# One block, three stages: Strassen's seven products for the channel mixing of an attention and mixer block

## The reference

```python
def _moe2_ref(x, w_tok1, w_tok2, w_ch1, w_ch2):      # the part that is changed
    xt = x.transpose(0, 2, 1)
    h = np.maximum(xt @ w_tok1, 0.0) @ w_tok2        # token mixing, 576 -> 256 -> 576
    u = x + h.transpose(0, 2, 1)
    h2 = np.maximum(u @ w_ch1, 0.0) @ w_ch2          # channel mixing, 512 -> 1536 -> 512
    return (u + h2).astype(np.float32)

def reference(...):
    attn_out = _attn_ref(...)                        # 8 heads, windows of 32 keys, plain or dilated by 4
    x = attn_out.transpose(0, 2, 1, 3).reshape(B, S, H * D)
    x = _moe_ref(x=x, ...)                           # shift mix, relu squared, sigmoid gate
    return _moe2_ref(x=x, ...)
```

## Time and profile before

| what | value |
|---|---|
| median of 3 runs | 696.34 us (695.63 to 697.08) |
| the profiled execution, span from first to last instruction | 694.4 us |
| the profiled execution's own time | not given apart from its span; the median lies 1.9 us above the span |
| TensorE busy (PE) | 686.7 us, 99% |
| VectorE (DVE), ScalarE (ACT), GpSimd (POOL) busy | 362.6, 230.6 and 201.7 us |
| mean granted clock of TensorE | 0.997 |
| first matmul of the mixer | 335.6 us |
| DMA | 181493 packets, 47.23 MB |

### The profile page before, as it was taken

How to read it: one execution, slowest core, us unless ns; L and a number is a source line. 1 busy time by engine, 2 the same in 40 slices (tenths; PEclk the granted TensorE clock), 3 DMA queues, 4 the chain that set the end, 5 groups by cost and what they waited for, 6 DMA issues and landing times.

```text
span 694.4 us, 15537 instructions
## 1 busy us (share of the span) xinstructions
PE 686.7 (99%) x6377; PEld 613.1 (88%) x6377; DVE 362.6 (52%) x635; ACT 230.6 (33%) x516; POOL 201.7 (29%) x249
## 2 busy tenths in 40 slices
PE   8999999999999999999999999999999999999997
PEld 7879999999999999999888879888788888888886
DVE  5579877676868668586752145221462125311121
ACT  4573653536353554546421122111231122111110
POOL 6574646546464645453072000000000000000000
PEclk9999999999999999999999999999999999999999
DMA  9972243233423331343630310403122221300011
GB/s 202 227 183 47 52 80 79 44 65 71 88 43 65 56 79 38 82 68 119 246 58 14 59 43 34 68 13 64 61 35 34 43 35 60 64 6 0 1 61 30
DMA packets 181493, 47.23 MB, mean 68 GB/s; under 512 B 168360, under 2 KB 173872, under 8 KB 181424
## 3 DMA queue, kind: packets, MB, share of 16 engines
q1 hardware_dynamic: 172448, 40.82, 26.9%
q10 hardware_dynamic: 8976, 5.43, 3.1%
HBM read 31.53 MB, written 4.72 MB: 52 GB/s over the span
## 4 chain that ended last, share of the span: by engine, by line
PE 97%; ACT 1%; DVE 1%; POOL 0%; issue 0%; DVEq 0%; POOLq 0%; ACTq 0%
PE bank L968 13%; PE bank L970 12%; PE bank L969 12%; PE tq L968 8%; PE tq L970 8%; PE tq L969 8%; PE s L1574 4%; PE s L1573 4%; PE s L1572 4%; PE bank L1573 3%; PE bank L1574 3%; PE bank L1572 3%; PE bank L844 3%; PE bank L1023 2%; PE s L632 2%; PE bank L768 1%
## 5 line engine op out<-in xcount | busy, mean ns | idle before, releaser
L1564 DVE SCALAR_TENSOR_TENSOR h_lo<-bank,h_hi 128x512 fp32r<-128x512 f32 (+1 forms) x30 | 18.9, 637 | 100.7 <-ACT h_hi L1558 100.6
L1564 DVE SCALAR_TENSOR_TENSOR h_lo<-tq,h_hi 128x512 fp32r<-128x512 f32 (+1 forms) x30 | 18.9, 636 | 99.0 <-ACT h_hi L1558 99.0
L1063 POOL TENSOR_TENSOR k_lo<-kr,k_hi 128x288 fp32r<-128x288 f32 x64 | 55.2, 866 | 25.6 <-ACT k_hi L1059 25.5
L1105 DVE RECIPROCAL rg<-rg 128x288 f32<-128x288 f32 x32 | 61.4, 1921 | 0.0
L1558 ACT ACTIVATE h_hi<-tq 128x512 fp32r<-128x512 f32 (+1 forms) x30 | 16.7, 556 | 118.7 <-PE bank L1574 97.0
L1558 ACT ACTIVATE h_hi<-bank 128x512 fp32r<-128x512 f32 (+1 forms) x30 | 16.7, 556 | 118.0 <-PE bank L1574 93.4
L968 PE MATMUL bank<-k_hi,WV_hi 128*128 128x288 f32 x184 | 55.5, 301 | 0.0
L969 PE MATMUL bank<-k_hi,WV_lo 128*128 128x288 f32 x184 | 54.3, 295 | 0.0
L970 PE MATMUL bank<-k_lo,WV_hi 128*128 128x288 f32 x184 | 54.1, 294 | 0.0
L1574 PE MATMUL s<-C_hi,h_lo 128*128 128x512 f32 x120 | 47.6, 396 | 0.0
L1572 PE MATMUL s<-C_hi,h_hi 128*128 128x512 f32 x120 | 47.1, 393 | 0.3 <-DVE urows L1601 0.3
(11 more groups left out here) (239 smaller groups left out, 1982.8 us busy)
## 6 DMA issues: line engine op xcount, KB each, us to landing
C_raw<-in_moe_w_ch SPq DMA_DIRECT2D x6, 1024.0 KB, 10.9
urows<-blocks SPq DMA_DIRECT2D x64, 64.0 KB, 2.1
out_x<-urows SPq DMA_DIRECT2D x16, 256.0 KB, 2.0
vt<-in_v SPq DMA_DIRECT2D x70, 48.0 KB
qraw<-in_q SPq DMA_DIRECT2D x128, 24.0 KB, 1.9
kraw<-in_k SPq DMA_DIRECT2D x128, 24.0 KB, 2.0
xraw<-blocks SPq DMA_DIRECT2D x48, 64.0 KB, 2.1
WK_raw<-in_moe_w_k SPq DMA_DIRECT2D x4, 512.0 KB, 6.1
```

The costliest lines, as they stand in the source:

```text
L1063: e.tensor_tensor(lo, t, hi.bitcast(F32), ALU.subtract).then_inc(Z.lo_done, 1)
L1105: e.reciprocal(t, t).then_inc(Z.r_done, 1)
L1564: e.scalar_tensor_tensor(lo, ps[:, 0:w], 0.0, hi.bitcast(F32), ALU.max, ALU.subtract).then_inc(Z.h2l_done, 1)
```

## The change

It replaces the four calls of `phase2_body` by three stages over all batches: `token_stage()`, `up_stage()`, `down_stage()`. Phase 1 stays, except that the channel weights are no longer loaded and split there: the turn of batch 1 (`x_blocks(1)`, `x_rows(1)`) and a first load of 1 MB are put there.

**Token stage.** The same products as before for each batch, the down products now as 48 matmuls of 288 columns. The low parts of x move from VectorE to GpSimd for batches 1 to 3. u is spilled to DRAM (`keep_u`), 1.2 MB for each batch. Beside it, w_ch1 is loaded in three slices; GpSimd forms Strassen's sums of its blocks (`w1_sums`), and of u's (`u_sums`).

**Up stage.** 24 steps q = 0 to 23, six for each batch. Each step makes two tiles of the hidden layer for all 576 positions, by seven half products (`half_product`) of six matmuls with 288 columns. Partial results are combined in PSUM by going on in the same bank, with a copy by ScalarE in between, and by three adds on VectorE. The hidden tiles (four blocks of 128x288, 0.59 MB for a step) are stored to DRAM.

**Down stage.** 84 chunks, 21 for each batch (7 products of 3 chunks), 12 matmuls of 288 columns each. The hidden layer is loaded back (3.5 MB for each batch), GpSimd and VectorE form the sums, ScalarE and VectorE split each chunk. Output comes with the channels on the partitions; VectorE transposes 32x32 blocks, and the stores to DRAM write rows of 128 bytes.

```diff
         def x_parts(b, i):
...
-            return dict(scalar=scalar, vector=vector)
+            return dict(scalar=scalar, gpsimd=lows) if b else dict(scalar=scalar, vector=lows)
...
         def x_blocks(b, d):
...
+                elif b == 1:
+                    e.wait_ge(Z.mm_done, HP * NU - DT)
+                    e.wait_ge(Z.lo_done, FT1 * NU)
+                    e.wait_ge(Z.x2_done, 4 * DT)
                 else:
+                    e.wait_ge(Z.mm_done, HP * NU)
                     e.wait_ge(Z.x2_done, DT * NU)
+                    if b == 3:
+                        e.wait_ge(Z.xt_in2, XT_IN)
...
         def phase1():
...
-            ff[-8].append(load_channel_weights())
-            ff[-3].append(split_weights2(N_T))
+            ff[-8].append(load_w1(0))
             for d in range(DT):
                 ff[d // 2 - 32].append(x_blocks(0, d))
+                ff[d // 2 - 6].append(x_blocks(1, d))
             ff[-31].append(x_rows(0))
+            ff[-4].append(x_rows(1))
...
+        def token_stage():
+            steps = [x_parts(1, i) for i in range(NTT)] + [x_blocks(2, d) for d in range(DT)] + [x_rows(2)]
+            steps += [token_up(0, m) for m in range(2)] + [w1_sums(0)] + token_rows(0)
+            steps += [x_parts(2, i) for i in range(NTT)] + [keep_u(0)] + [x_blocks(3, d) for d in range(DT)] + [x_rows(3)]
+            steps += [token_up(1, m) for m in range(2)] + token_rows(1) + [u_sums(0), load_w1(1), keep_u(1)]
+            steps += [x_parts(3, i) for i in range(NTT)] + his(w1[0]) + los(w1[0])
+            steps += [token_up(2, m) for m in range(2)] + his(u0) + token_rows(2) + [keep_u(2)] + los(u0)
+            steps += [w1_sums(1)] + [token_up(3, m) for m in range(2)] + token_rows(3) + [keep_u(3), load_w1(2)]
+            steps += his(w1[1]) + [w1_sums(2), u_sums(1)]
+            return steps
...
+        def up_step(q):
...
+            def tensor(e):
...
+                    half_product(e, q, A11, a).then_inc(Z.p1_done, 1)
+                    half_product(e, q, S1, sum_c).then_inc(Z.p5_done, 1)
+                    half_product(e, q - 1, A22, sums_a[(q - 1) % 2], onto=True).then_inc(Z.p4_done, 1)
+                e.wait_ge(Z.c1_copied, q + 1)
+                half_product(e, q, S2, a, onto=True).then_inc(Z.p6_done, 1)
+                half_product(e, q, A12, sum_b).then_inc(Z.p2_done, 1)
+                half_product(e, q, S4, sum_c, onto=True).then_inc(Z.p3_done, 1)
+                half_product(e, q, S3, a, onto=True).then_inc(Z.p7_done, 1)
...
+        def up_stage():
+            extra[0] += [w1[1][i][1] for i in range(4)]
+            extra[1] += [w1[1][i][1] for i in range(4, 7)]
+            extra[2] += [x for i in range(4) for x in w1[2][i]]
+            extra[3] += [x for i in range(4, 7) for x in w1[2][i]]
+            for m in range(7):
+                extra[4 + m // 4] += u_parts(1, m)
...
+            last = NJ * (B - 1)
+            extra[last] += [load_w2(0), w2_sums(0)]
+            extra[last + 1] += [load_h(0), w2_parts(0)]
+            extra[last + 2] += [load_w2(1), w2_sums(1), w2_parts(1), w2_parts(2)]
+            extra[last + 3] += [chunk_parts(0), chunk_parts(1)]
+            extra[last + 4] += [load_w2(2), w2_sums(2), w2_parts(3), w2_parts(4)]
+            for q in range(NQ + 1):
+                steps += [up_step(q)] + extra[q]
```

More of the change, by code:

```diff
@@ new lines, in build @@
+        W1, o = [], R0
+        for s in range(NSL):
+            ops = []
+            for i in range(7):
+                w, o = weights(f"W1_{s}_{i}_", [P, 2 * SL], o)
+                ops.append(w)
+            W1.append(ops)
+        xT1, _ = weights("xT1", [P, NTT * DM], R0 + NSL1)
+        h1, o_ = split("h1", [P, 2 * DM], R0 + 2 * NSL1)
+        xT3, _ = weights("xT3", [P, NTT * DM], o_)
+        xTs = [xT0, xT1, xT0, xT3]
+        xblocks1 = at("xblocks1", [P, DT * S], F32, o_)
+        U0 = o
@@ new lines, in build @@
+        U = []
+        for m in range(2):
+            ops = []
+            for i in range(7):
+                w, o = weights(f"U{m}_{i}_", [P, 2 * HALF], o)
+                ops.append(w)
+            U.append(ops)
+        U1 = U0 + 56 * 2 * HALF
+        xblocks2 = at("xblocks2", [P, DT * S], F32, U1)
+        HQ0 = o
+        hq = [at(f"hq{i}", [P, 4 * HALF], F32, o + 16 * HALF * i) for i in range(NHQ)]
+        o += 16 * HALF * NHQ
+        SPARE = o
+        W2, o = [], 0
+        for i in range(7):
+            if i == 3:
+                o = R0
+            w, o = weights(f"W2_{i}_", [P, NJ * 2 * P], o)
+            W2.append(w)
@@ L1320, in x_dst @@
         def x_dst(b):
[L1321 removed]
+            t = (xblocks0, xblocks1, xblocks2, xblocks2)[b]
+            return t[:, 0:XS * P], t[:, XS * P:DT * S]
         def x_blocks(b, d):
@@ L1408, in part @@
             def part(t, c):
                 return t[:, DM * m + c[0]:DM * m + c[1]]
[L1411 to L1412 removed]
             def tensor(e):
                 if m == 0:
[L1416 to L1421 removed]
+                    for m_ in range(2):
+                        work_free(e, b, m_)
@@ new lines, in keep_u, with sync, load_w1 @@
+        def keep_u(b):
+            def sync(e):
+                e.wait_ge(Z.u_done, 8 * (b + 1))
+                e.dma_start(ud[b], X[:, b * XB:(b + 1) * XB].rearrange("p (d n) -> p d n", d=DT)[:, :, 0:S])\
+                    .then_inc(Z.u_kept, 16)
+            return dict(sync=sync)
+        A11, S1, S2, A12, S3, S4, A22 = range(7)
+        B11, T1_, T2_, B21, T3_, B22, T4_ = range(7)
+        w1_in = (Z.w1_in0, Z.w1_in1, Z.w1_in2)
+        def load_w1(s):
+            def sync(e):
+                if s == 0:
+                    e.wait_ge(Z.mm_done, HP * NU - DT)
+                    e.wait_ge(Z.lo_done, FT1 * NU)
+                elif s == 1:
+                    e.wait_ge(Z.t1p_done, 4)
+                else:
+                    e.wait_ge(Z.t2p_done, 8 * B)
+                for i, kh, fh in ((S3, 0, 1), (A22, 1, 1), (A11, 0, 0), (A12, 1, 0)):
+                    f0 = NJ * P * fh + SL * s
+                    e.dma_start(tiles(W1[s][i][2][:, :], 2), kview(w_ch1)[:, 2 * kh:2 * kh + 2, f0:f0 + SL]).then_inc(w1_in[s], 16)
+            return dict(sync=sync)
@@ L1694, in main @@
             run(name, e, phase1())
-            for b in range(B):
-                run(name, e, phase2_body(b, last=b == B - 1))
+            run(name, e, token_stage())
+            run(name, e, up_stage())
+            run(name, e, down_stage())
         N_MASKS_P = 4 + 10
```

768 lines of the change are left out of this document (468 added, 300 removed).

## The result

The changed kernel takes **765.14 us** (median of 4 runs, 759.9 to 773.0) beside 696.71 us for the kernel before on the same chip, a ratio of 1.095 (1.090 to 1.100). The forecast was 730.5 with a range up to 750: the sign was right, the size was not. The execution that was profiled took 759.94 us with a span of 758.1.

What follows compares the result with a forecast made beforehand. TensorE's matmul time was taken as the bound, busy 99%. From 694.4, less 35.0 for matmuls, plus 47.5 token, 18.5 up, 2.2 down and 1.0 tail gave 728.6 of span; 1.9 more made 730.5 us, range 712 to 750.

Steps and rivals of the forecast that it cites:

- The chain of the token stage: Token stage: x's row DMAs, 22.2 us of SP's queue each turn, cause three waits; stage 100.3 against 52.8 us, plus 47.5.
- the wait of 19.0: Token stage, batch 0: relu stands behind batch 1's splits, so token down starts at 361.1 in place of 342.1.
- Rival 1: Token stage, SP's queue: the turns are never late, so faster, 682 us with all the stage's waits hidden; chance 0.06.
- The matmul distance: All three stages: matmuls of 288 columns start 0.1329 us apart; in channel mixing 267.9 against 302.9 us, gain 35.0.
- The wait at step 20: Up stage: ScalarE waits for GpSimd's two sums of w_ch2 ahead of step 20's copies; TensorE waits 8.3 us.
- GpSimd's low parts and sums ... fit between: Token stage: GpSimd's low parts (1.3 us each) and sums (about 1.3 for 512 columns) fit between, adding no wait.
- 28.1 us, free as long as three chunks of lead cover the order: Down stage: VectorE's 28.1 us of work for each batch hides behind 33.5 us of matmuls.
- in the first batch ... 2.2 us: Down stage, first batch: GpSimd's sums come behind w_ch2's last two (7 us), costing 2.2 us.
- gaps of PE along the down stage: Down stage: TensorE gaps all along it were named as one sign that the forecast would be wrong.
- Rival 3: VectorE bounds the down stage: splits 20% longer beside GpSimd's sums, 3 to 5 us each batch, 743 to 750; chance 0.15.
- The third wait of the token stage: Token stage, before batch 3's token down: x rows, then ScalarE's splits of x and w_ch1, relu and low part; 17.0 us.
- 1.7 us behind each long wait: Token and up stages: six us at a granted clock of 0.72 lose 1.7 us, taken once behind each long wait.

Runs made afterwards that it cites:

- two_queues: Changed kernel with nearly the reordered token list of list_order, and 12 of each turn's 32 DMAs issued from ScalarE's queue; 735.0 us, 1.055 of the kernel before.
- list_order: Changed kernel with only the token stage's list reordered, the splits of the next batch's x behind the relu; 752.0 us, 1.079 of the kernel before.
- all_moved: Changed kernel with two_queues, up_order, block sums on VectorE, x low parts back on VectorE and a buffer for the third turn; 696.4 us, 0.999 of the kernel before.
- thin_sums: Changed kernel with GpSimd's sums of w_ch2 and h made over one column only, output wrong; 742.8 us, 1.066 of the kernel before.
- up_order: Changed kernel with the up stage's side work in another order and one more wait on GpSimd; 746.5 us, 1.068 of the kernel before.
- idle_sums: Fastest kernel (690.0 us) plus nine unneeded GpSimd additions on a scratch tensor for each batch of the down stage; 700.7 us, 1.005 of the kernel before.

## Why the prediction missed

**Right.** The chain of the token stage: "x_rows(1) takes SP until 354.6" (352.1), the wait of 19.0 (16.7), that of 7.6 (7.2), and the ends through ACT by the splits of x. two_queues shows that the issue time of the queue is the cause, list_order that the list's order adds to it. Rival 1, with issuing small and all waits hidden, would have had the stage at 51.6 us; it took 104.6. The matmul distance held: 134 us for 1008 matmuls in the up stage once its waits were gone (138.8 in all_moved with 3.1 of waits), and 136.2 in thin_sums' down stage. The wait at step 20 was found and sized at 8.3, measured 10.0. thin_sums (3.4 left) shows that the length of GpSimd's two sums holds most of it, up_order (2.9 left) that starting them a step earlier hides them.

**Wrong, the step.** "GpSimd's low parts and sums ... fit between", and in the down stage "28.1 us, free as long as three chunks of lead cover the order" with "in the first batch ... 2.2 us". Each engine's load was added up by itself, and the price of two engines meeting was put at nothing. GpSimd's 73.2 us in the down stage are partly VectorE's too: DVE is busy 137.5 us there, 89%, where 4 x 28.1 is 112 and thin_sums has 100.5. The prediction's own sign of being wrong, gaps of PE along the down stage, came true. Rival 3 named the right engine, but priced the neighbour at "20% more" for a split, a figure that no row gives; and its 33.7 takes 20% of all 28.1 us, where 20% of the splits alone gives 31.4. What it held against the rival, that DVE is "this full" in phase 1, was not so: DVE is busy 73% there on average (245.8 of 335.5 us), and the stage asked for 84%. Measured is 2.6 times as long beside a sum of h and over 5 times beside one of w_ch2, for the operation that meets it. Its 3 to 5 us for each batch, 12 to 20 in all, hold the 18.0 by which the stage missed, but by luck: the batches behind the first last 35.75 us (689.42 less 653.66) against 33.5, 2.25 more each, and the first 13.3 more, where the sums of w_ch2 stand. The 18.0 are 8.8 of waits, 6.0 of clock and 3.2 that are mostly edges of waits; thin_sums gives back 17.8.

**The same term in the other stages.** The third wait of the token stage was 21.8, not 17.0. The prediction ended it through ACT, behind seven high parts of w_ch1 (4.3 us; they took 3.7), and left VectorE's seven low parts, which stand ahead of h's on that engine, out of the chain. They took 11.75 us beside GpSimd, where seven take 4.29 alone, and ended last, although x had landed about 5 us sooner than forecast. At step 2 of the up stage three low parts took 4.66 in place of 2.1, and the wait was 5.1, not 2.6.

**Clock, mis-sized.** The prediction took 1.7 us behind each long wait, 6.8 in all; the clock cost 17.0. Behind the waits of 16.7 and 10.0 us it was 1.5 and 1.7, as forecast; behind those of 7.2 and 21.8 it was 2.5 and 2.7, and 2.6 behind the one of 5.1 at step 2, for which the prediction took none. The largest part is the down stage's first batch: from 606.4 to 620.0, with waits of 4.8, 0.5 and 0.5 us up to 614.6, the clock stayed at the lower level and cost 6.0. Short waits don't do this everywhere. The later batches' waits of 1.3 us cost no clock, and idle_sums' down stage has 14.8 us of waits, none over 2.3, at a granted clock of 1.00 throughout. Another 5 us are mostly the edges of the waits, a term that the prediction doesn't have.

**Time against span.** The prediction added 1.9 us. The profiled execution has 1.8, but it was the fastest of four, and the median lies 5.2 higher. Of the 34.6 us by which the forecast missed, 29.5 are in the span, and the others are this spread, whose cause no run here looked for.

## What to carry to other kernels

Before work moves from VectorE to GpSimd, look at its operands. If VectorE's neighbouring operations read two SBUF tensors, each GpSimd operation that reads SBUF takes up to its own length from VectorE: here a sum that takes VectorE 0.75 us took up to 1.2 us of it when GpSimd made it, and putting all of them back made the stage shorter although VectorE was the fullest engine beside TensorE. Add up the two engines as one where such operations meet, and put GpSimd's beside PSUM reads. And when work loses its cover, count DMA issues, not bytes: 32 small ones are 22 us of a queue, and a second queue and a relu ahead of them in the list gave back 28 us. Strassen's saving in matmul time was real all along (134 us for 1008 matmuls, in both stages); with order, queues and engines set right, some 7 of its 35 us remain (690.0 beside 697.2).

## What the runs showed of the hardware

- VectorE with two SBUF inputs against GpSimd on unrelated tensors: 0.75 us becomes 1.70 (sum of 1.15), 1.22 (copy of 0.67), 1.97 (sums of h back to back), 3.97 (sums of 1536 columns). Both lose: GpSimd's sum goes from 1.15 to 1.59 or 1.9. VectorE's PSUM adds stay at 0.44 to 0.46.
- One DMA issue costs its queue 0.64 to 0.75 us on SP and on ScalarE alike, in parallel; SP's 16 took 10.55 us beside ScalarE's queue and 10.26 without.
- The granted clock read 0.50 while TensorE stood for 17 us, and 0.67 over the first four microseconds in which it worked again; it stayed at 0.50 from 606.4 to 620.0 although TensorE was busy 11.95 of these 13.65 us.
